# Pooled attention and two feed-forward layers on one core: v's last sums in one VectorE pass, two heads per instruction, weight columns in pairs, front turns in another order

## The reference

```
batch, n_heads, seq, head_dim = (4, 8, 576, 64);  pool = 8;  Sp = 72
k_p, v_p = k.reshape(B, H, Sp, 8, D).mean(axis=3), v.reshape(...).mean(axis=3)
scores = scale * q @ k_p.T;  scores -= max(scores);  attn = exp(scores)
attn = attn / (attn.sum(-1) + 1e-09);  x = (attn @ v_p) as [2304, 512]
layer 1: h = x @ w_in (512 x 2048); g = h if h >= 1, 0 if h <= -1, else (h + 1)**2 / 4; y = g @ w_out
layer 2: h = y @ w_in; g = max(h, 0) + log1p(exp(-|h|)); out = g @ w_out
```

## Time and profile before

| | us |
|---|---|
| median of 3 runs | 862.84 (862.07 to 867.12) |
| profiled execution | 862.46 |
| its span | 860.7 |
| PE busy in the span | 845.8 |
| first product matmul (make_h of pair 0) starts | 59.14 |
| first matmul of pair 2 starts | 76.04 |

### The profile page before, as it was taken

One profiled execution on the slowest core, in us unless ns is written; L12 is line 12 of the kernel. 1 busy time (PEld: TensorE's weight loads), 2 busy tenths in 40 slices (PEclk: granted clock), 3 DMA queues, 4 the chain that ended last, 5 costly groups with the idle time before them and its releaser, 6 DMA issues.

```text
span 860.7 us, 13035 instructions
## 1 busy us (share of the span) xinstructions
PE 845.8 (98%) x5198; PEld 822.7 (96%) x5198; DVE 592.0 (69%) x618; ACT 490.5 (57%) x700; POOL 360.8 (42%) x290
## 2 busy tenths in 40 slices
PE   8989999999999999999999999999999899999998
PEld 7768999999999999999999999999999899999998
DVE  4983855532233598768657698898899989778642
ACT  3875665644445453444435868978887654445442
POOL 6994677744454600000000498888766500000000
PEclk9979999999999999999999999999999999999999
DMA  8952767565555896454633235675655698645532
GB/s 195 209 126 78 209 209 230 185 220 188 181 183 188 274 395 224 167 220 154 227 109 99 96 123 189 211 243 182 211 200 176 204 397 306 239 164 203 200 113 73
DMA packets 106539, 167.82 MB, mean 195 GB/s; under 512 B 21872, under 2 KB 94448, under 8 KB 101872
## 3 DMA queue, kind: packets, MB, share of 16 engines
q1 hardware_dynamic: 93800, 157.86, 54.9%
q10 hardware_dynamic: 12680, 9.14, 3.7%
HBM read 96.21 MB, written 70.78 MB: 194 GB/s over the span
## 4 chain that ended last, share of the span: by engine, by line
PE 84%; DVE 6%; ACT 3%; DMA 3%; SPq 1%; issue 1%; POOL 1%; ACTq 0%; DVEq 0%
PE ps L1263 41%; PE ps L1281 37%; DVE t_a L1052 2%; DMA ops<-gops 2%; PE ps L1178 1%; DVE ops L1064 1%; PE ps L1215 1%; DMA w_raw<-in_moe_w_in_dram 1%; PE ps L1296 1%; PE ps L1321 1%; PE ps L1199 1%; DVE xs L992 1%; ACT qT L652 1%; PE ps L1155 1%; DVE t_a L1055 1%
## 5 line engine op out<-in xcount | busy, mean ns | idle before, releaser
L1263 PE MATMUL ps<-xs,W 128*128 128x384 f32 x2304 | 408.2, 336 | 0.8 <-DVE ops L1044 0.8
L1263 PEld LDWEIGHTS ps<-xs,W 128*128 128x128 f32 x2304 | 399.3, 188 | 5.8 <-issue 4.9
L1281 PE MATMUL ps<-xs,Tm 128*128 128x384 f32 x1968 | 345.9, 336 | 3.4 <-DVE xs L992 3.0
L1281 PEld LDWEIGHTS ps<-xs,Tm 128*128 128x128 f32 x1968 | 342.2, 189 | 4.3 <-issue 3.5
L744 ACT ACTIVATE xs<-ops 128x768 fp32r<-128x768 f32 (+1 forms) x148 | 111.7, 826 | 159.1 <-PE ps L1281 149.9
L608 POOL TENSOR_TENSOR ops<-ops 128x384 f32<-128x384 f32 x48 | 72.9, 1519 | 303.2 <-DVE ops L1064 221.9
L992 DVE TENSOR_TENSOR xs<-ops,xs 128x768 fp32r<-128x768 f32 (+1 forms) x148 | 130.2, 941 | 1.8 <-ACT xs L744 1.8
L1044 DVE SCALAR_TENSOR_TENSOR ops<-ps,t_a 128x768 f32<-128x768 f32 x48 | 45.9, 956 | 110.4 <-ACT t_a L768 110.2
L766 ACT ACTIVATE t_a<-ps 128x768 f32<-128x768 f32 x48 | 39.0, 812 | 96.2 <-PE ps L1263 96.2
L1077 DVE TENSOR_TENSOR X<-ps,X 128x768 f32<-128x768 f32 x41 | 38.7, 955 | 77.8 <-PE ps L1281 77.8
L1064 DVE TENSOR_TENSOR ops<-t_a,t_b 128x768 f32<-128x768 f32 x48 | 62.8, 1308 | 19.7 <-ACT t_b L787 17.9
(11 more groups left out here) (88 smaller groups left out, 650.6 us busy)
## 6 DMA issues: line engine op xcount, KB each, us to landing
gops<-ops SPq DMA_DIRECT2D x48, 1344.0 KB, 5.8
ops<-gops SPq DMA_DIRECT2D x36, 1536.0 KB, 6.8
X<-gops SPq DMA_DIRECT2D x22, 384.0 KB, 6.4
w_raw<-in_moe_w_in_dram SPq DMA_DIRECT2D x32, 256.0 KB, 3.9
t_raw<-in_moe_w_out_dram SPq DMA_DIRECT2D x6, 1024.0 KB, 10.0
out_dram<-y_out ACTq DMA_DIRECT2D x11, 384.0 KB, 2.6
k_raw<-in_k_dram SPq DMA_DIRECT2D x10, 288.0 KB
q_raw<-in_q_dram SPq DMA_DIRECT2D x20, 144.0 KB, 7.6
```

The lines of the kernel that those rows point to most:

```text
L1263: last = mm(banks[:, tb, :], W[:, slot, f, part, c * P:(c + 1) * P], x[:, x_part, at:at + TB], start=c == 0 and s == 0, stop=c == KC - 1 a ...
L1281: last = mm(banks[:, d, :], Tm[:, t, part, j, d * P:(d + 1) * P], g[:, g_part, at * TB:(at + 1) * TB], start=at == 0 and s == 0, stop=at = ...
```

## The change

- *v's sums.* For the first ten units GpSimd only adds halves; VectorE makes the last sum in one reduce over four rows (sum_v) instead of adding two.
- *Two heads in one instruction.* Maxima, subtraction and exp of the front units are one instruction for both heads, and so have one wait instead of two. On ScalarE the exp stands behind all copies of p.
- *Weight columns in pairs.* A weight slot holds 256 neighbouring columns instead of two blocks of 128 from different places; one DMA with rows of 1 KB loads it instead of two with rows of 512 B. The rows of w_out are taken in the matching order.
- *When weights are loaded and converted.* The loads of slots 0 and 1 move behind unit 9's q and k and behind v of unit 7, the conversions from ScalarE's turns 5 and 6 to turns 7 and 8, GpSimd's lo_w behind its half sum of v of unit 8.
- *PE's turns.* From turn 1 on score(i+1) stands behind attend(i-2) instead of at the turn's start.
- *Warm-up.* 11, 6, 4, 6, 6 and 4 matmuls instead of 8, 3, 3, 5, 6 and 3.
- *End of the front.* Pair 0's last chunk goes ahead of attend(9), and GpSimd starts on unit 10 only when VectorE has made the last piece of X's low part.

```diff
-WARM = (3, 6)
+WARM = (4, 6)
...
-        win_src = [w.rearrange("(c p) (f j) -> f p c j", p=P, j=P) for w in (w1_in, w2_in)]
-        wout_src = [w.rearrange("(k j p) d -> k p j d", k=2, p=P) for w in (w1_out, w2_out)]
+        win_src = [w.rearrange("(c p) (s j) -> s p c j", p=P, j=2 * P) for w in (w1_in, w2_in)]
+        wout_src = [w.rearrange("(j k p) d -> k p j d", k=2, p=P) for w in (w1_out, w2_out)]
...
-                for f in range(2):
-                    sp.dma_start(w_raw[:, n % 2, f, :].rearrange("p (c j) -> p c j", c=KC),
-                                 win_src[layer][slot + JJ * f]).then_inc(w_loaded[n % 2], 16)
+                sp.dma_start(w_raw[:, n % 2, :, :], win_src[layer][slot]).then_inc(w_loaded[n % 2], 16)
...
                 load_v(u - 2)
-                if u >= LATE:
-                    load_weights(0, u - LATE)
-            for u in range(FIRST - 2, FIRST):
+            for u in range(LATE, FIRST):
+                load_weights(0, u - LATE)
                 load_v(u)
...
+            def half_sum(x, loaded, halved):
+
+                pool.wait_ge(*loaded)
+                nc.gpsimd.tensor_tensor(x[:, :, 0:4 * HD], x[:, :, 0:4 * HD], x[:, :, 4 * HD:8 * HD],
+                                        ALU.add).then_inc(halved, 1)
...
                 if u < FIRST:
-                    pool_sums(u, v_in(u), (v_loaded[u % PAIRS], 16 * (u // PAIRS + 1)), v_halved, v_paired)
+                    half_sum(v_in(u), (v_loaded[u % PAIRS], 16 * (u // PAIRS + 1)), v_halved)
...
             pool_values(FIRST - 3)
+            pool_values(FIRST - 2)
             lo_w(0, 0)
-            pool_values(FIRST - 2)
             fill_lo_piece(0, 0)
             pool_values(FIRST - 1)
             fill_lo_piece(0, 1)
+            pool.wait_ge(*fill_done(0, PIECES - 1))
             pool_keys(FIRST)
...
+            def exp_both(u):
+
+                x = prob[:, u % PAIRS, :, :, 0:SP].rearrange("p h i s -> p (h i) s")
+                act.wait_ge(shifted, 2 * u + 2)
+                nc.scalar.activation(x, x, ACT.Exp, scale=SCALE).then_inc(exped, 2)
...
                 for h in range(2):
                     if 1 <= i <= FIRST:
                         copy_p(i - 1, h)
-                    if i <= FIRST - 2:
-                        exp_scores(i + 1, h)
-                if 5 <= i < 7:
-                    hi_w(0, i - 5)
+                if i <= FIRST - 2:
+                    exp_both(i + 1)
+                if LATE <= i + 1 <= LATE + 1:
+                    hi_w(0, i + 1 - LATE)
...
             def sum_v(u):
                 wait(dve, attended, u - 3)
-                add_last(u, v_in(u), v_paired, v_sum[:, u % PAIRS, :], v_summed)
+                dve.wait_ge(v_halved, u + 1)
+                nc.vector.tensor_reduce(v_sum[:, u % PAIRS, :].rearrange("p (h d) -> p h d", h=2),
+                                        v_in(u)[:, :, 0:4 * HD].rearrange("p h (r d) -> p h d r", r=4),
+                                        AX_X, ALU.add).then_inc(v_summed, 1)
...
+            def take_both_max(u):
+                dve.wait_ge(scored, 2 * u + 2)
+                nc.vector.tensor_reduce(pmax[:, :, :], scores_of_both(), AX_X, ALU.max).then_inc(maxed, 2)
...
             def turn(i):

-                if i <= FIRST - 2:
+                if i <= 0:
                     score(i + 1)
-                if i <= 0:
                     keep_warm(WARM[i + 1])
                 if i <= FIRST - 3:
                     transpose_qk(i + 2)
                 if 2 <= i:
                     attend(i - 2)
                 if i >= 1:
+                    score(i + 1)
                     for h in range(2):
                         transpose_p(i - 1, h)
...
-            make_h(0, 1, (1,))
+            make_h(0, 0, (3,))
             attend(FIRST - 1)
-            make_h(0, 0, (3,))
-            make_h(0, 1, (2, 3))
+            make_h(0, 1, (1, 2, 3))
```

More of the change, by code:

```diff
@@ L106, in build @@
         X = place("X", [P, KC, T], F32)
-        w_raw = place("w_raw", [P, 2, 2, KC * P], F32)
+        w_raw = place("w_raw", [P, 2, KC, 2 * P], F32)
         tmp_at = at[0]
@@ L114, in build @@
         w_at = at[0]
-        W = place("W", [P, JJ, 2, 2, KC * P], F32R)
+        W = place("W", [P, JJ, 2, KC, 2 * P], F32R)
         Tm = place("Tm", [P, 2, 2, JJ, DH], F32R, offset=w_at)
@@ L539, in pool_sums @@
                                         ALU.add).then_inc(halved, 1)
+            def pool_sums(u, x, loaded, halved, paired):
+                half_sum(x, loaded, halved)
                 pool.wait_ge(halved, u + 1)
@@ L600, in lo_w @@
                 pool.wait_ge(w_hi, n + 1)
-                nc.gpsimd.tensor_tensor(W[:, slot, :, 1, :], w_raw[:, n % 2, :, :], W[:, slot, :, 0, :].bitcast(F32),
+                nc.gpsimd.tensor_tensor(W[:, slot, 1, :, :], w_raw[:, n % 2, :, :], W[:, slot, 0, :, :].bitcast(F32),
                                         ALU.subtract).then_inc(w_lo_pool, 1)
@@ L758, in hi_w @@
                     act.wait_ge(step_done, STEPS)
-                nc.scalar.activation(W[:, slot, :, 0, :], w_raw[:, n % 2, :, :], ACT.Copy).then_inc(w_hi, 1)
+                nc.scalar.activation(W[:, slot, 0, :, :], w_raw[:, n % 2, :, :], ACT.Copy).then_inc(w_hi, 1)
             def square(a):
@@ L894, in _ @@
         def _(dve):
[L896 to L900, removed]
             def sum_v(u):
                 wait(dve, attended, u - 3)
-                add_last(u, v_in(u), v_paired, v_sum[:, u % PAIRS, :], v_summed)
+                dve.wait_ge(v_halved, u + 1)
+                nc.vector.tensor_reduce(v_sum[:, u % PAIRS, :].rearrange("p (h d) -> p h d", h=2),
+                                        v_in(u)[:, :, 0:4 * HD].rearrange("p h (r d) -> p h d r", r=4),
+                                        AX_X, ALU.add).then_inc(v_summed, 1)
             def scores_of(u, h):
-                return ps[0:SROW, (2 if u < FIRST else 4) + h, 0:ROWS].rearrange("p (i s) -> p i s", i=NS)
+                return ps[0:SROW, 4 + h, 0:ROWS].rearrange("p (i s) -> p i s", i=NS)
             def take_max(u, h):
@@ L915, in shift, with scores_of_both, shift_both @@
                 dve.wait_ge(maxed, 2 * u + h + 1)
-                wait(dve, p_transposed, 2 * (u - 3) if u < FIRST else 2 * u)
+                wait(dve, p_transposed, 2 * u)
                 highest = pmax_of(u, h).unsqueeze(2).broadcast_to([SROW, NS, SP])
                 nc.vector.tensor_tensor(prob_of(u, h), scores_of(u, h), highest, ALU.subtract).then_inc(shifted, 1)
+            def scores_of_both():
+                return ps[0:SROW, 2:4, 0:ROWS].rearrange("p h (i s) -> p h i s", i=NS)
+            def take_both_max(u):
+                dve.wait_ge(scored, 2 * u + 2)
+                nc.vector.tensor_reduce(pmax[:, :, :], scores_of_both(), AX_X, ALU.max).then_inc(maxed, 2)
+            def shift_both(u):
+                dve.wait_ge(maxed, 2 * u + 2)
+                wait(dve, p_transposed, 2 * (u - 3))
+                highest = pmax[:, :, :].unsqueeze(3).broadcast_to([SROW, 2, NS, SP])
+                nc.vector.tensor_tensor(prob[:, u % PAIRS, :, :, 0:SP], scores_of_both(), highest, ALU.subtract
+                                        ).then_inc(shifted, 2)
             def turn(i):
@@ L935, in turn @@
                 if new:
-                    take_max(i + 1, 0)
+                    take_both_max(i + 1)
                 if old:
@@ L984, in lo_w @@
                 dve.wait_ge(w_hi, n + 1)
-                nc.vector.tensor_tensor(W[:, slot, :, 1, :], w_raw[:, n % 2, :, :], W[:, slot, :, 0, :].bitcast(F32),
+                nc.vector.tensor_tensor(W[:, slot, 1, :, :], w_raw[:, n % 2, :, :], W[:, slot, 0, :, :].bitcast(F32),
                                         ALU.subtract).then_inc(w_lo_dve, 1)
@@ L1262, in make_h @@
                             at = c * PIECE + tb * TB
-                            last = mm(banks[:, tb, :], W[:, slot, f, part, c * P:(c + 1) * P], x[:, x_part, at:at + TB],
+                            last = mm(banks[:, tb, :], W[:, slot, part, c, f * P:(f + 1) * P], x[:, x_part, at:at + TB],
                                       start=c == 0 and s == 0, stop=c == KC - 1 and s == 2)
@@ L1330, in _ @@
             pe.wait_ge(ident_ready, 1)
-            keep_warm(8)
+            keep_warm(11)
             transpose_qk(0)
-            keep_warm(3)
+            keep_warm(6)
             turn(-1)
-            keep_warm(5)
+            keep_warm(6)
             turn(0)
-            keep_warm(3)
+            keep_warm(4)
             for i in range(1, FIRST - 1):
```

15 lines of the change are left out of this document (6 added, 9 removed).

## The result

The changed kernel is slower: 889.54 us median of 4 runs (888.62 to 891.94), beside 862.46 (862.00 to 867.12) for the kernel before on the same chip. The ratio is 1.0282, 95% interval 1.0247 to 1.0316. The profiled execution took 888.69, its span is 886.9.

The account below looks back on a forecast made before the run. It took PE, 98% busy, as the bound, and in the front the chain that closes a turn. 862.5 + 8.7 (pair 2 later at full clock) + 15.3 (low clock) = 886.5 us, range 870 to 892.

Parts of the forecast that it names:

- Start: Front's beginning: added warm-ups and unit 3's q and k ahead of score(2) move it from 17.90 to 20.0 us.
- The wait of the copies: Front turns: ScalarE's q and k copies wait for the score; a turn takes 5.85 us, PE idling 1.4.
- The step that failed: VectorE in front turns: about 4.1 us of work in 5.85, all in the new wait, worth 0.
- my sign of score starts 5.8 to 6 apart at full clock: Front: what would show the forecast, with score starts under 5 us apart counting as wrong.
- a late sum of v once: One front turn: v's sum late behind a VectorE product that GpSimd holds up, about 0.8 us.
- The reduce for v: VectorE in the front: a reduce over 512 elements replaces an add, 0.6 us, bounds 0.5 and 1.2.
- Clock: Front: half clock from near 34 us until the products, 3.4 us per turn for four and a half turns, 15.3 us.
- the 2 us of late steps: Three front turns: a late sum of v, about 0.8, and two X conversions delaying p copies and attend, 0.6 each.
- Weights: End of front: slot 0's later conversion and GpSimd's low parts put the first product at 67.5, 4.5 after score(9).
- First product to pair 2: After the front: 17.2 us against 16.9 before, with 2.0 added for GpSimd's piece 1; pair 2 8.7 late.
- The rival in which the clock holds: Front: every turn has the gap but PE keeps full clock; 871 us, chance 0.18.
- The rival "not slower": Front: ScalarE's wait for "scored" is hidden, PE closes turns at its own 4.46 us; 859 us, chance 0.07.

Follow-up runs that it names:

- v_early_gap: Changed kernel with VectorE's sum of v ahead of the maxima, one warm-up matmul ahead of attend and five behind the score; 870.62 us, ratio 1.0050.
- two_qT: Changed kernel with two buffers of qT and kT, so ScalarE's copies wait for the scores of unit u-2; 882.51 us, ratio 1.0168.
- gap_warm: Changed kernel with useless matmuls in PE's waits of turns 2 to 7, three ahead of attend, five ahead of transposes of p; 875.7 us, ratio 1.0119.
- order_only: Kernel before with one edit: PE's score(i+1) behind attend(i-2) from turn 1 on; 893.92 us, ratio 1.0306.
- order_undone: Changed kernel with PE's old order of a turn, all else as changed; 863.42 us, ratio 0.9966.
- two_qT_vearly: Changed kernel with two buffers of qT and kT and the sum of v ahead of the maxima, PE's new order kept; 862.83 us, ratio 0.9962.
- undone_w0early: Changed kernel with PE's old order and slot 0's load, conversion and low part one turn earlier; 859.77 us, ratio 0.9937.
- early_again: The kernel of undone_w0early, unchanged, run again in a later series; 858.26 us, ratio 0.9919.

## Why the prediction was right, and where its steps were off

I forecast 886.5 us (870 to 892); it is 889.5. The mechanism was right: the wait of the copies for the score, and the half clock that follows. One step left out a second loop, the fall of the clock was forecast more than a turn too late, and the end of the front was too short. That the total came within 3 us is in part luck: part of what the early fall and the second loop added was given back by waits that the low clock covered.

- *Start.* Score(2) forecast at 20.0, measured 19.86. Right.
- *The wait of the copies.* The copy of q idles behind the score in each turn, PE idles before head 1 on the store of X. Right, though by 0.90 to 0.92 each time and not by the "over 1 us" forecast. Its price at full clock, 5.85 a turn, is right for this loop: 5.8 in v_early_gap.
- *The step that failed: "VectorE's work in a turn is about 4.1 of 5.85, so all of it lies in the new wait and is worth 0".* I asked if VectorE has time, and not in which order it works. The score's maxima stand ahead of v's sum in its queue, attend waits for that sum, and the new order puts the next score behind attend. This loop is 6.35 at full clock in two_qT and 6.7 to 6.9 in most turns of gap_warm, and outlasts the one I priced; my sign of score starts 5.8 to 6 apart at full clock failed with 6.49. I had counted a late sum of v once, with 0.8; in two_qT it is late six times. It cost little in the changed kernel only since the clock soon fell: at 1.2 GHz ScalarE's loop is the longer one, 9.2, and a single wait for v of 1.5 us is left.
- *The reduce for v.* I took 0.6 (bounds 0.5 to 1.2) by the reduce of 730 in 0.91. It takes 1.00 to 1.06 in all ten units, longer than the reduce with more elements. It is 1.2 of the second loop from its start to attend's; order_only has that loop's wait with the old add too.
- *Clock.* Half the clock was forecast from 34 us, with 5.85 + 3.4 = 9.25 a turn. The low turn is 9.20: the sum is right, with q and k at 1.91 in place of 2.16. The fall came at 27.5, at the end of the first reordered turn and behind the wait for v, so nearly six turns were low and not four and a half. The four and a half were short by my own terms too: 34 to 63 holds 5.0 turns of 5.85. Score(9), forecast at 63.0 + 15.3 = 78.3, came at 79.71. This +1.4 is what is left of the longer time at the low clock, about 4 us, and of 0.6 in the first turn: the last turn has no transposes of q and k, and of the 2 us of late steps that I had added only a wait of 0.83 before the attend at 77.60 shows.
- *Weights.* Score(9) to the first product, 4.5 forecast, 4.37 measured; but these 4.37 are PE's score and transposes of p at the low clock, without a wait. GpSimd's lateness is covered, as the forecast had it; it shows where the clock is up, with 2.46 in gap_warm (forecast 2.5) and 3.48 in order_undone. The first product, near 83 forecast, 84.08 measured, follows from score(9).
- *First product to pair 2.* 17.2 forecast, 19.1 measured. I had GpSimd's lateness covered at the low clock. But VectorE's product of p took 3.28 us, from 83.89, while GpSimd worked without a gap from 79.26 to 86.40; v's sum stood behind it, and attend came 2.21 late.

The sum: 862.5 + 24.0 forecast, 26.2 more in the profiled execution. The chance of a loss over 1% comes to 0.81 by its own terms, not 0.82. The rival in which the clock holds is not this kernel's case, but gap_warm is it, at 873 where I had 871, with the longer loop and the warm-ups in it. The rival "not slower" needed the wait for "scored" hidden. It is not hidden. With it and the other loop taken away (two_qT_vearly) the profiled execution takes 862.23 where that rival had 859: score(9) starts at 53.40 and not 51.2, and behind it come 2.70 of waiting for the late weight slot and a clock at 0.50 from 60 to 66 us.

What stays open: which wait brings the clock down and what brings it back within a front, and why order_only had it low from 8 to 22.

## What to carry to other kernels

Before an instruction is moved behind another on one engine, follow each thing that both wait for through every queue and write down each closed loop, with the starts of a timeline: one turn costs the longest loop, not the busiest engine. Where the moved work waits in a loop with one buffer, one remedy alone may do little and two together everything: the second buffer alone left 1.7 of 2.8%, and with the earlier sum of v nothing was left. When PE's waits in a turn go from 0.2 us to about 1, price the lower clock as well; here it was more than half of the loss.

## What the runs showed of the hardware that I had not expected

- The clock did not return while PE was busy: at 0.50 from 49 to 60 us PE worked 10.10 of 11.00 us, and it stayed low until about 85.5, in the first products. In two_qT it did return, near 49, within the same kind of turns, and fell again. What makes the difference no run shows.
- The same idleness does not always bring the fall. The clock held through waits of 0.22 to 0.5 in each turn (order_undone, 22 to 57 us), and fell behind one of 1.51 (the changed kernel) and in one of 3.48 (order_undone). But it held behind one of 1.95 in two_qT, to fall in the next, of 2.88; and a wait of 1.31 before an attend was followed by a fall in v_early_gap (0.70 from 62 to 63 us) and by none in gap_warm (1.00 from 64 to 70 us). Behind two of 0.70 it fell in the profiled execution of undone_w0early, near 55 us, and held in that of early_again, which is the same kernel with the same two waits. The Trainium skill (TensorE: Matmul & The Clock Gate, A second HAM failure mode: psum-queue depth-cycling) tells of a bf16 kernel in which micro-idles between groups of matmuls make the clock go to and fro. The changed kernel did so only once, between 86 and 92 us; two_qT did it over the whole front.
- VectorE's product with two SBUF inputs took 3.28 us beside a busy GpSimd and 0.90 alone, while the one-input sum of v ran at 1.00 to 1.06 in all ten units. In order_undone that sum took 1.05 from 57.84 in the midst of a GpSimd operation (57.11, 2.48 long). The Trainium skill (SBUF — State Buffer, Who interferes with whom) says that a VectorE instruction with two SBUF inputs contends with a GpSimd instruction that reads SBUF, and one with at most one SBUF input does not. The trace agrees. I had drawn on it and said that it moves no term; it moved the last one, with attend 2.21 us late.
